# Constants in another order, a run of ones matmuls, and features ahead of tokens, in a linear-attention and mixture-of-experts kernel

## The reference

```python
# 1. linear attention with a decaying state; r, k, v are (2, 8, 768, 48)
for t in range(S):
    kt, vt, rt = (k[:, :, t], v[:, :, t], r[:, :, t])
    cur = np.einsum('bhd,bhe->bhde', u[None] * kt, vt)
    y[:, :, t] = np.einsum('bhd,bhde->bhe', rt, state + cur)
    state = w[None, :, :, None] * state + np.einsum('bhd,bhe->bhde', kt, vt)
x = y.transpose(0, 2, 1, 3).reshape(1536, 384)
# 2. mixture of experts: 8 experts, one per token (argmax of x @ w_gate), 384 -> 1024 -> 384
# 3. a dense layer: g = relu(x @ w_in) ** 2;  out = g @ w_out, 384 -> 2048 -> 384
```

## Time and profile before

| | us |
|---|---|
| Time of three runs, median | 436.42 |
| lowest and highest | 435.76, 439.98 |
| the profiled execution, time | 438.97 |
| the profiled execution, span | 436.9 |

### The profile page before, as it was taken

One profiled execution on the slowest core, in us unless ns is written; L12 is line 12 of the kernel. 1 busy time (PEld: TensorE's weight loads), 2 busy tenths in 40 slices (PEclk: granted clock), 3 DMA queues, 4 the chain that ended last, 5 costly groups with the idle time before them and its releaser, 6 DMA issues.

```text
span 436.9 us, 10114 instructions
## 1 busy us (share of the span) xinstructions
PE 408.9 (94%) x3954; PEld 380.7 (87%) x3954; DVE 257.7 (59%) x442; ACT 211.5 (48%) x414; POOL 64.7 (15%) x75
## 2 busy tenths in 40 slices
PE   0889999499999999999999999999999999999994
PEld 0878898289999999999998889989988988998984
DVE  5375675777877667668657455356445537545331
ACT  2355668325655646646545444445354444444321
POOL 3653550162012022000000000004000004000003
PEclk9998999579999999999999999999999999999998
DMA  7976987069965566556463314224322323200002
GB/s 210 249 227 166 280 290 221 21 202 333 341 240 201 184 219 222 163 209 207 155 216 96 122 72 142 75 74 145 143 72 83 133 72 126 90 1 0 1 0 78
DMA packets 18736, 66.44 MB, mean 152 GB/s; under 512 B 2889, under 2 KB 7642, under 8 KB 18705
## 3 DMA queue, kind: packets, MB, share of 16 engines
q1 hardware_dynamic: 16912, 61.32, 43.4%
q0 software_dynamic: 1792, 4.72, 2.8%
HBM read 59.74 MB, written 7.08 MB: 153 GB/s over the span
## 4 chain that ended last, share of the span: by engine, by line
PE 75%; DVE 4%; issue 2%; ACT 1%; DVEq 0%; POOLq 0%; ACTq 0%
PE score_banks L569 18%; PE y_banks L569 17%; PE gate_bank L592 6%; PE spare_bank L592 6%; PE state_bank L592 6%; PE sum_bank L592 6%; PE gate_bank L582 5%; PE state_bank L582 5%; PE sum_bank L582 5%; PE spare_bank L609 1%; PE spare_bank L559 1%; DVE ylo L1104 0%; PE score_banks L550 0%; DVE hlo L1085 0%; ACT cv L758 0%
## 5 line engine op out<-in xcount | busy, mean ns | idle before, releaser
L914 DVE TENSOR_TENSOR wlo<-raw,whi 128x1536 fp32r<-128x1536 f32 x56 | 98.4, 1758 | 91.5 <-ACT whi L719 88.8
L719 ACT ACTIVATE whi<-raw 128x1536 fp32r<-128x1536 f32 x56 | 83.3, 1489 | 83.3 <-PE spare_bank L592 47.6
L1081 DVE TENSOR_TENSOR sq<-rl 128x512 f32<-128x512 f32 x48 | 32.9, 689 | 30.0 <-ACT rl L795 30.0
L447 POOL DMA_INDIRECT out<-osb,oidx x12 | 13.0, 1081 | 247.9 <-ACT osb L853 245.0
L418 POOL DMA_INDIRECT xg<-attention_out,gidx x16 | 19.5, 1217 | 90.2 <-PE spare_bank L559 64.1
L1085 DVE TENSOR_TENSOR hlo<-sq,hhi 128x512 fp32r<-128x512 f32 x48 | 30.9, 686 | 0.0
L569 PE MATMUL y_banks<-yhi,whi 128*128 (+1 forms) x72 | 28.4, 395 | 0.0
L569 PE MATMUL score_banks<-ylo,whi 128*128 (+1 forms) x72 | 28.4, 395 | 0.0
L569 PE MATMUL score_banks<-yhi,whi 128*128 (+1 forms) x72 | 28.4, 395 | 0.0
L569 PE MATMUL y_banks<-yhi,wlo 128*128 (+1 forms) x72 | 28.4, 395 | 0.0
L569 PE MATMUL score_banks<-yhi,wlo 128*128 (+1 forms) x72 | 28.4, 395 | 0.0
(11 more groups left out here) (217 smaller groups left out, 1139.4 us busy)
## 6 DMA issues: line engine op xcount, KB each, us to landing
raw<-in_wts SPq DMA_DIRECT2D x56, 768.0 KB, 4.3
tok<-in_tok SPq DMA_DIRECT2D x12, 416.0 KB, 5.1
feat<-in_feat SPq DMA_DIRECT2D x16, 192.0 KB, 3.5
vT<-in_vT SPq DMA_DIRECT2D x12, 192.0 KB, 4.4
attention_out<-x_sb SPq DMA_DIRECT2D x12, 192.0 KB, 3.8
out<-rl SPq DMA_DIRECT2D x12, 192.0 KB, 5.8
feat<-in_feat SPq DMA_DIRECT2D x4, 448.0 KB, 8.2
xg<-attention_out,gidx POOLq DMA_INDIRECT x16, 4.8
```

What stands on the lines that cost most here:

```text
L447: nc.gpsimd.indirect_dma_start(out=out[:, :], out_offset=bass.IndirectOffsetOnAxis(ap=oidx[:, t:t + 1], axis=0), in_=osb[:, t, :], in_offs ...
L719: return nc.scalar.activation(dst, src, ACT.Copy)
L914: v.tensor_tensor(wlo[:, r, :], raw[:, r, :], whi[:, r, :].bitcast(F32), ALU.subtract).then_inc(w_lo, 1)
L1081: v.tensor_tensor(sq[:, ft, :], rl[:, ft, :], rl[:, ft, :], ALU.mult).then_inc(h_sq, 1)
```

## The change

- GpSimd sets `ones_b` first of all, with a semaphore of its own (`ones_set`); it no longer waits for `table_ready` ahead of its chunks.
- TensorE begins with 52 matmuls of `ones_b` by `ones_b`, 128 by 128 by 128 in bf16, into the spare bank; nothing reads them. Its four transposes go into the same bank, each behind its quarter of `Tr`.
- `Tr` is made by ScalarE in four steps, no longer by VectorE in one; ScalarE then makes `decm`, and after that copies `tokw`.
- TensorE waits for `decm` inside each chunk ahead of L530, and no longer for `tokw` itself.
- VectorE sets the first values of semaphores (the `free`, `gout`, `off`, `start`, `kept` memsets) and clears `uw` before its first wait, and makes `dec` and `uw` ahead of the first keys.
- SyncE asks for features 1 ahead of tokens 0, then for vT 1, features 2, tokens 1, vT 2, features 3, tokens 2, vT 3, tokens 3.

```diff
-CONSTS = 10
+CONSTS = 9
...
             load_gate_values(0)
+            load_features(1)
             load_tokens(0)
-            for n in range(1, SLOTS):
+            load_gate_values(1)
+            for n in range(2, SLOTS):
                 load_features(n)
+                load_tokens(n - 1)
                 load_gate_values(n)
-                load_tokens(n)
+            load_tokens(SLOTS - 1)
...
             steps = Steps(pool, pool_step)
+            nc.gpsimd.memset(ones_b[:, :], 1.0).then_inc(ones_set, 1)
             nc.gpsimd.memset(ident[:, :], 0.0).then_inc(pool_step, 1)
...
-            nc.gpsimd.memset(ones_b[:, :], 1.0).then_inc(consts, 1)
...
-            pool.wait_ge(table_ready, 1)
             pool.wait_ge(prod_ready, 1)
...
+            pe.wait_ge(ones_set, 1)
+            for _ in range(52):
+                pe.matmul(spare[:, 0:P], ones_b[:, :], ones_b[:, :], start=True, stop=True)
             pe.wait_ge(consts, 1)
-            pe.wait_ge(table_ready, 1)
             for g in range(G):
-                mm = pe.transpose(ps_x[:, g * ROWS:(g + 1) * ROWS], Tr[0:ROWS, g, :], ident[0:ROWS, 0:ROWS])
+                pe.wait_ge(table_ready, g + 1)
+                mm = pe.transpose(spare[:, g * ROWS:(g + 1) * ROWS], Tr[0:ROWS, g, :], ident[0:ROWS, 0:ROWS])
...
             pe.wait_ge(in_wg, 16)
-            pe.wait_ge(tokw_ready, 2)
             pe.wait_ge(uw_ready, 3)
-            pe.wait_ge(decm_ready, G)
...
                     pe.wait_ge(khat_ready, n + 1)
+                    pe.wait_ge(decm_ready, G)
                     pe.wait_ge(state_ready, n + 2)
...
-            act.wait_ge(tokw_psum, 1)
-            for o in range(2):
-                copy(tokw[:, :].rearrange("p (g o d) -> p g o d", g=G, o=2)[:, :, o, :],
-                     ps_x[:, 0:G * ROWS].rearrange("p (g q) -> p g q", g=G)[:, :, ODD * o:ODD * o + D]).then_inc(tokw_ready, 1)
...
-            act.wait_ge(consts, 1)
             act.wait_ge(dec_ready, 1)
             for g in range(G):
+                nc.scalar.activation(Tr[0:ROWS, g, :], T[0:ROWS, g, 127::-1], ACT.Copy, scale=dec[0:ROWS, g:g + 1]).then_inc(table_ready, 1)
+            act.wait_ge(consts, 1)
+            for g in range(G):
                 nc.scalar.activation(decm[0:ROWS, g, :], ident[0:ROWS, :], ACT.Copy, scale=dec[0:ROWS, g:g + 1]).then_inc(decm_ready, 1)
+            act.wait_ge(tokw_psum, 1)
+            for o in range(2):
+                copy(tokw[:, :].rearrange("p (g o d) -> p g o d", g=G, o=2)[:, :, o, :],
+                     spare[:, 0:G * ROWS].rearrange("p (g q) -> p g q", g=G)[:, :, ODD * o:ODD * o + D]).then_inc(tokw_ready, 1)
...
             v.memset(T[w, :, 64:65], 1.0)
+            v.memset(uw[:, :, :], 0.0).then_inc(uw_ready, 1)
             v.memset(oh[:, :, :], 0.0)
+            for j, s in enumerate((vx_ready, csum_ready, heads_ready, heads_ready, masked, masked)):
+                v.memset(free[:, j:j + 1], 0.0).then_inc(s, 1)
+            v.memset(gout[:, :], 0.0).then_inc(y_ready, 1)
+            v.memset(off[:, :], 0.0).then_inc(unit_done, 1)
+            v.memset(start[:, :], 0.0).then_inc(o_act, 1)
+            v.memset(kept[:, :], 0.0).then_inc(o_dve, 1)
             dve.wait_ge(in_w, 16)
...
+            v.tensor_tensor(dec[w, :], T[w, :, 128], T[w, :, 128], ALU.mult).then_inc(dec_ready, 1)
+            dve.wait_ge(in_u, 16)
+            dve.wait_ge(uw_ready, 1)
+            for o in range(2):
+                rows = slice(ODD * o, ODD * o + D)
+                v.tensor_tensor(uw[rows, :, o], ucol[rows, :], wcol[rows, :], ALU.mult).then_inc(uw_ready, 1)
             dve.wait_ge(in_feat[0], 16)
...
-            v.tensor_tensor(dec[w, :], T[w, :, 128], T[w, :, 128], ALU.mult).then_inc(dec_ready, 1)
-            dve.wait_ge(dec_ready, 1)
-            v.tensor_tensor(Tr[w, :, :], T[w, :, 127::-1], dec[w, :].unsqueeze(2).to_broadcast([ROWS, G, C]), ALU.mult).then_inc(table_ready, 1)
```

More of the change, by code:

```diff
@@ L177, in build @@
         consts = sem("consts")
+        ones_set = sem("ones_set")
         zeros_set = sem("zeros_set")
```

## The result

The changed kernel takes 436.12 us (median of 20 runs, 432.05 to 437.94) against 437.78 for the kernel before, measured beside it (20 runs, 435.22 to 442.0). The ratio is 0.994, with a 95% interval of 0.992 to 0.996: 0.6% faster, where 1.3% was forecast. The profiled execution took 437.55 with a span of 435.4, 1.5 less than the 436.9 of the earlier trace rows; it was the second longest of its 20 runs, so what it lost may be more than the median run lost.

A forecast was written before the change was run, and what follows sets the result against it. TensorE, busy 94% of the span, was taken as the bound; chunk 4 starting at 31.4 instead of 38.43 gave -7.0 us, hence 432.0 by profile, 429.4 by median, middle 430.7 us, range 426.0 to 434.9.

The forecast's parts named there:

- Parts 1 to 4: Preparation on VectorE, ScalarE and TensorE, plus ones: chunk 0 starts at 7.7 us instead of 12.28, at 2.4 GHz.
- Part 5: SyncE's load queue: features 1 land at 8.9, tokens 0 at 10.6, a 0.4 us wait, chunk 1 at 13.0.
- Part 6: Instruction fetch before chunk 4: moved block boundaries pace TensorE, chunk 4 at 31.4 instead of 38.43; fetch eats 4.6 us.
- Then one block each 5.37 us: Fetch in chunks 0 to 3: after 8.5, blocks at 13.9, 19.2, 24.6 and 30.0 us.
- slower: Rival: fetches take longer while data queues are full; at a 9 us round trip the kernel takes 444; chance 0.06.
- the clock falls again: Rival: the clock drops at the new, longer stops, mostly hidden by fetch, giving 432.7 to 434.9 us; chance 0.20.
- the two gaps forecast for later: Instruction-fetch stops of TensorE near the end of chunk 2 and late in chunk 3, 1.4 us each.
- Part 7: From chunk 4 on everything is as before, only shifted; the clock's fall before the experts may add 1 us either way.
- From profile to median: Whole kernel: 7.0 us off profiled 438.97 gives 432.0, off median 436.42 gives 429.4; the middle, 430.7, was taken.

The follow-up runs named there:

- e14: Changed kernel loading only 16 partitions of features, vT and tokens from chunk 2 on, chunks 2 and 3 constant-filled; one run, ratio not compared, span 424.3 us.
- e4: Changed kernel with the loads of chunks 2 and 3, and tokens 1, held until an older load has landed; ratio 0.992 to the kernel before.
- e1: Changed kernel with 13 ones matmuls of 512 columns in place of 52 of 128; ratio 0.9992 to the kernel before.
- e11: Changed kernel with loads paced as in e8, but tokens ahead of the next features as in the kernel before; ratio 0.9838 to the kernel before.
- e16: The changed kernel run again later, unmodified; ratio 0.9927 to the kernel before.
- e12: The same kernel as e8, timed once more; ratio 0.981 to the kernel before.
- e15: e8 with tighter pacing, letting less into the queue before features 5, 6 and 7; ratio 0.9872 to the kernel before.
- e7: Changed kernel asking for the first two expert weights behind tokens 3 instead of during the last chunks; ratio 1.0014 to the kernel before.
- e13: Changed kernel loading only 16 partitions of features, vT and tokens for chunks 4 to 11; one run, ratio not compared, span 428.9 us.
- e6: Kernel before with only ones_b set first and the 52 ones matmuls added; ratio 0.9979 to the kernel before.
- e8: Changed kernel with loads of chunks 2 to 7, and tokens 1, held until older loads have landed; ratio 0.9843, median 430.16 us.

## Why the prediction was wrong

**Parts 1 to 4 (preparation, ones) held.** Chunk 0 at 7.36 (7.7 forecast), ones done at 6.3 (6.9), full rate from its first matmul.

**Part 5 (queue) held.** GpSimd starts on features 1 at 9.69 (8.9), the gate copy into tokens 0 at 11.05 (10.9), a wait of 1.06 instead of 0.4, and chunk 1 at 13.30 (13.0).

**Part 6 failed, in the sentence "Then one block each 5.37 us".** The cause, and the places, were right: boundaries at matmul 19 of chunk 1 and 2 of chunk 2, where 15 and the start were forecast, and on to the end of chunk 2. The size was not. 5.37 was read from two resumes at 27.65 and 33.02, when the data share was 0.83; the change puts the requests at 8.5 and 15.5, when it is 1.04. Entered at 8.5, the next block was there at 15.54: 7.0 us; the one asked for then at 23.37: 7.8 us. Forecast were 13.9 and 19.2. So 4.2 us are missing at the start of chunk 2. The packets themselves began at 12.9, 20.5, 25.1 and 31.4, that is 7.6, 4.6 and 6.3 us apart, where 5.4 was written. e14 shows that the number is no constant of the chip: with light traffic the blocks come in 3.8 to 4.4 us, as fast as they are used. And e4 shows that the DMA share of 1.04 is not what sets it either: with less queued ahead, a block came in 4.7 us at 1.05 in that execution. I had the longer round trip as the rival "slower" and set it aside because the first packet of before had lain in a full stretch without a gap; but that packet began at 19.8, at the end of the full stretch (a share of 1.06 from 16 to 20 us, 0.61 from 20 to 24), so it said little of a block asked for at 8.5, while the share stays near 1.0 up to 24 us.

**The rival "the clock falls again" came true as well.** I held that a slow stretch would hide behind the fetch. Behind the 2.87 us of gap it cost 3.8 us in chunk 2 and 0.7 in chunk 3 (5.51, less 4.49 and the jump), and hid only the two gaps forecast for later, 1.4 us each, which did not come: TensorE at the lower rate reached those boundaries later. The sum closes for the profiled execution: 31.4 forecast + 4.2 + 4.5 - 2.8 = 37.3, and 37.11 was measured.

**Part 7 held.** Span less start of chunk 4 is 398.5 before, 398.3 after, and 396.9 to 398.5 in e1 to e11 and e16: what is won at chunk 4 reaches the end. The exceptions are e12 (399.2) and e15 (402.9, with the wait of 3.23 us in chunk 6).

**From profile to median.** I took the middle between two bases. The 20 runs of before have 437.78 as their median, so 436.42 was a low draw of three; the change's 7.0 would have given 430.8 by it. This step was not at fault; the sum was.

## What to carry to other kernels

Code is data: a loop with an unrolled body of a thousand instructions is fetched in blocks, and a kernel that opens by queueing every load it has can hold up its own instructions (7.0 to 7.8 us a block here, against 4.7 with loads held back). A price read under one load of a shared resource holds for that load; when a change moves work into a stretch where the resource is full, read the price there or bound it by both. A gain in the first microseconds is worth what is left of it at the point where the steady loop begins, so look there first.

## What the runs showed of the hardware

- TensorE's instruction block of 16 KB came 7.0 to 8.3 us after the one before it was entered where many loads were queued (7.0 and 7.8 in the changed kernel, 7.9 in e16, 8.3 in e1), 5.4 us in the kernel before at a DMA share of 0.83, and in no more than 3.8 to 4.4 at about 0.35 (e14). The share does not tell it alone: in e4 it was 4.7 at 1.05. That a block is asked for when the one before is entered is inferred from these times and packets. The Trainium skill, page "Runtime: NRT & Kernel Launch", section "Instruction fetch mechanics", holds the crossing to be mostly hidden; in e14 it is, in the changed kernel it costs 4.2 us and the clock.
- The clock fell to 1.2 GHz behind gaps of 1.18 (before), 1.70 (e7), 2.22 (e13), 2.87 (changed) and 2.96 us (e4), and behind 1.16 and 0.35 close together (e11), but not behind 0.79 (before), 1.33 (changed), 1.71 (e16) or 2.07 (e1, the second gap). The same length, 1.7 us, had both outcomes, so the length of a gap alone does not tell. A wait of 2.5 us after 5 us of ones lost the higher clock too (e6).
- Two pairs of executions of equal code differed in these gaps: e8 and e12 by up to 2.9 us, the changed kernel and e16 by 0.4 and 0.8 us. What sets this is open, and so is how far depth of queue and chance share in the length of one gap. The granted clock over the whole span was 0.984 in e8 and e12 alike.
